# The first expert's rows gathered by token number, and its two products ahead of the end of the scatters

## The reference

```python
x = attn_out.transpose(0, 2, 1, 3).reshape(B * S, H * D)   # 2304 tokens x 512
do_compute = (x @ w_skip) > 0
xc = x[do_compute]
logits = xc @ w_gate                                       # 8 experts
e_idx = np.argmax(logits, axis=1)
gate_w = softmax(logits)[np.arange(len(xc)), e_idx]
for e in range(8):
    mask = e_idx == e
    h = np.maximum(xc[mask] @ w1[e], 0.0)                  # 512 -> 1024
    y[mask] = gate_w[mask, None] * (h @ w2[e])             # 1024 -> 512
out[do_compute] = xc + y
h = out @ w_in                                             # 512 -> 2048
g = where(h >= 1, h, where(h <= -1, 0, (h + 1)**2 / 4))
return g @ w_out                                           # 2048 -> 512
```

## Time and profile before

| | us |
|---|---|
| median of 3 runs | 693.38 |
| lowest, highest | 689.04, 693.66 |
| the profiled execution, device time | 696.19 |
| its span from first to last instruction | 694.3 |
| busy: TensorE, DVE, ACT, POOL | 639.6, 313.7, 188.2, 126.8 |

### The profile page before, as it was taken

One profiled execution on the slowest core, in us unless ns is written; L12 is line 12 of the kernel. 1 busy time (PEld: TensorE's weight loads), 2 busy tenths in 40 slices (PEclk: granted clock), 3 DMA queues, 4 the chain that ended last, 5 costly groups with the idle time before them and its releaser, 6 DMA issues.

```text
span 694.3 us, 12370 instructions
## 1 busy us (share of the span) xinstructions
PE 639.6 (92%) x5133; PEld 552.5 (80%) x5133; DVE 313.7 (45%) x570; ACT 188.2 (27%) x361; POOL 126.8 (18%) x135
## 2 busy tenths in 40 slices
PE   6888880699999999899999999999999999999995
PEld 3766660599999999788888888888888888888994
DVE  3766250051212111575545555456554565545652
ACT  1545450141111111122223322233222332223331
POOL 1333117002222223883000200002000020000201
PEclk8999695699999999999999999999999999999998
DMA  8687295883777885231000100001000010000100
GB/s 272 199 272 243 95 363 214 291 305 110 261 266 270 276 277 187 78 107 30 1 1 0 61 1 0 1 0 60 0 0 0 0 60 0 0 0 1 61 1 31
DMA packets 39476, 76.34 MB, mean 110 GB/s; under 512 B 3079, under 2 KB 17844, under 8 KB 38916
## 3 DMA queue, kind: packets, MB, share of 16 engines
q1 hardware_dynamic: 36556, 66.26, 27.9%
q0 software_dynamic: 2880, 9.52, 3.6%
HBM read 65.83 MB, written 9.94 MB: 109 GB/s over the span
## 4 chain that ended last, share of the span: by engine, by line
PE 86%; issue 4%; DMA 4%; DVE 3%; SPq 2%; POOL 1%; ACT 0%; DVEq 0%
PE pair L1025 28%; PE pair L1038 16%; PE bank L1038 13%; PE pair L982 11%; PE out_pair L992 5%; PE bank L992 5%; DMA k_loc<-kT 2%; PE out_pair L884 2%; PE pair L842 2%; PE bank L862 1%; PE out_pair L923 1%; DMA k_str<-kT 1%; DVE yl L780 1%; PE bank L966 1%; PE pair L836 1%
## 5 line engine op out<-in xcount | busy, mean ns | idle before, releaser
L1025 PE MATMUL pair<-yh,WIH 128*128 128x512 f32 (+1 forms) x320 | 116.7, 371 | 0.2 <-ACT yh L589 0.2
L1025 PE MATMUL pair<-yh,WIL 128*128 128x512 f32 (+1 forms) x320 | 116.6, 371 | 0.0
L613 ACT ACTIVATE cl<-cl,half 128x512 f32<-128x512 f32 (+1 forms) x80 | 54.4, 681 | 186.8 <-DVE cl L801 186.8
L809 DVE TENSOR_TENSOR gl<-gr,gh 128x512 fp32r<-128x512 f32 (+1 forms) x80 | 54.1, 677 | 73.6 <-ACT gh L622 73.2
L801 DVE TENSOR_SCALAR cl<-pair 128x512 f32<-128x512 f32 (+1 forms) x80 | 51.0, 637 | 72.9 <-PE pair L1025 72.9
L508 POOL DMA_INDIRECT out<-XT,tok x18 | 19.2, 1066 | 351.0 <-DVE XT L789 347.0
L1025 PE MATMUL pair<-yl,WIH 128*128 128x512 f32 (+1 forms) x320 | 79.6, 369 | 1.7 <-DVE yl L780 1.7
L982 PE MATMUL pair<-xw,WE 128*128 128x168 f32 x512 | 75.5, 309 | 0.0
L982 PEld LDWEIGHTS pair<-xw,WE 128*128 128x128 f32 x512 | 74.4, 192 | 0.1
L622 ACT CAST gh<-gr 128x512 fp32r<-128x512 f32 (+1 forms) x80 | 46.3, 579 | 86.1 <-PE bank L1038 61.0
L1025 PEld LDWEIGHTS pair<-yh,WIH 128*128 128x128 f32 x320 | 60.6, 189 | 11.3 <-ACT yh L589 0.6
(11 more groups left out here) (142 smaller groups left out, 804.8 us busy)
## 6 DMA issues: line engine op xcount, KB each, us to landing
WE<-w SPq DMA_DIRECT2D x16, 2048.0 KB, 10.0
xrow<-x_sorted SPq DMA_DIRECT2D x6, 781.5 KB, 9.7
v_loc<-vl SPq DMA_DIRECT2D x4, 1024.0 KB, 7.5
raw_in<-win SPq DMA_DIRECT2D x16, 256.0 KB, 8.5
raw_out<-wout SPq DMA_DIRECT2D x16, 256.0 KB, 2.6
q_loc<-qT SPq DMA_DIRECT2D x4, 576.0 KB, 6.4
k_loc<-kT SPq DMA_DIRECT2D x4, 576.0 KB, 7.8
v_str<-vs SPq DMA_DIRECT2D x8, 256.0 KB, 4.6
```

The lines of the kernel that those rows point to most:

```text
L613: act.activation(cl[:, 0:n], cl[:, 0:n], ACT.Square, bias=half[:, :], scale=0.5).then_inc(squared, 1)
L809: dve.tensor_tensor(gl[:, f % 2, 0:n], gr[:, 0:n], gh[:, f % 2, 0:n].bitcast(F32), ALU.subtract).then_inc(g_low, 1)
L1025: last = pe.matmul(h2_b[f % 2][:, 0:tokens], w[:, c, P * f:P * (f + 1)], x[:, c, 0:tokens], start=(k == 0), stop=(k == 3 * DC - 1))
```

## The change

The rows of `xrow` are also written to HBM unsorted (`x_tokens`), by nine transfers from SP of two tiles each, as ACT finishes the tiles. DVE builds for each of the 18 tiles a table `hot`: for each of its tokens a 1 at the slot that the token has, among slots 0 to 167. TensorE multiplies these tables by the tile number and the row number of each token (36 small matmuls), which gives for each slot the token that belongs there; DVE makes of them `token_of`. POOL, after its first 4 scatters (`SCATTERS_FIRST`), waits until all nine writes are done (`rows_out`), gathers the first expert's 168 rows from `x_tokens` with two indirect transfers, and goes on with the other 14 scatters. SP loads only expert 1's rows from `x_sorted`.

`into(0)` and `outof(0)` now both stand ahead of the wait for expert 1's rows, and `into(1)` ahead of the sort. The result of expert 0 is copied out of PSUM by DVE (`y_first`), since the banks are needed. Expert 0's w1 is loaded before the last steps of attention (the attention tiles were moved to the other end of the shared space), and expert 1's w1 after the nine writes.

```diff
@@ sync @@
-            sp.wait_ge(pv_done, STEPS)
             load_w1(0, 0)
+            sp.wait_ge(pv_done, STEPS)
             load_w2(0, 0)
+            for t in range(0, NT, ROWS_OUT):
+                sp.wait_ge(rows_copied, t + ROWS_OUT)
+                sp.dma_start(xt[P * t:P * (t + ROWS_OUT)].rearrange("(t p) c -> p t c", p=P), xrow[:, t:t + ROWS_OUT, 0:D]).then_inc(rows_out, 16)
             load_w1(1, 1)
...
             sp.wait_ge(scattered, 16 * NT)
-            for par in range(2):
-                sp.dma_start(xfirst[:, 2 * par, :], xs[bass.ds(start_1 if par else 0, P), 0:D]).then_inc(first_in[par], 16)
-                sp.dma_start(xfirst[0:WIN - P, 2 * par + 1, :], xs[bass.ds(start_1 + P if par else P, WIN - P), 0:D]).then_inc(first_in[par], 16)
-
+            sp.dma_start(xfirst[:, 2, :], xs[bass.ds(start_1, P), 0:D]).then_inc(first_in[1], 16)
+            sp.dma_start(xfirst[0:WIN - P, 3, :], xs[bass.ds(start_1 + P, WIN - P), 0:D]).then_inc(first_in[1], 16)
+
+            sp.wait_ge(rows_out, 16 * (NT // ROWS_OUT))
@@ gpsimd @@
             for t in range(NT):
+                if t == SCATTERS_FIRST:
+
+                    pool.wait_ge(rows_out, 16 * (NT // ROWS_OUT))
+                    for r, rows_ in ((0, P), (1, WIN - P)):
+                        pool.wait_ge(tokens_ready, r + 1)
+                        pool.indirect_dma_start(xfirst[0:rows_, r, :], None, xt, bass.IndirectOffsetOnAxis(token_of[0:rows_, r:r + 1], 0)).then_inc(first_in[0], 16)
                 pool.wait_ge(rows_copied, t + 1)
@@ vector @@
+            dve.wait_ge(slot_f_in, 16)
+            dve.tensor_copy(slot_b[:, :], slot_f[:, :]).then_inc(slot_b_ready, 1)
...
             dve.tensor_copy(slot_of[:, :], posf[:, :]).then_inc(slots_ready, 1)
+
+            dve.wait_ge(slot_b_ready, 1)
+            for t in range(NT):
+                dve.tensor_scalar(hot[:, t, :], slot_b[:, 0:WIN], posf[:, t:t + 1], None, ALU.is_equal).then_inc(hot_ready, 1)
             link(dve.tensor_copy(starts[:, :], base[0:1, :, 0]))
             dve.sem_inc(starts_ready, 1)
+            for r, rows_ in ((0, P), (1, WIN - P)):
+                dve.wait_ge(token_ready, r + 1)
+                dve.tensor_copy(token_parts[0:rows_, r, :], token_b[r][0:rows_, 0:2]).then_inc(token_copied, 1)
+                dve.wait_ge(token_copied, r + 1)
+                dve.scalar_tensor_tensor(token_of[0:rows_, r:r + 1], token_parts[0:rows_, r, 0:1], float(P), token_parts[0:rows_, r, 1:2], ALU.mult, ALU.add).then_inc(tokens_ready, 1)
...
-                dve.tensor_copy(xw[:, par, :, 0:P], first_b[2 * par][:, :].rearrange("p (c n) -> p c n", c=DC)).then_inc(first_main, 1)
+                dve.tensor_copy(xw[:, par, :, 0:P], first_b[0][:, :].rearrange("p (c n) -> p c n", c=DC)).then_inc(first_main, 1)
+                if par == 0:
+
+                    for c in range(DC):
+                        dve.wait_ge(y_ready, c + 1)
+                        dve.tensor_copy(y_first[:, c, :], y_b[c][:, 0:WIN]).then_inc(y_kept, 1)
@@ tensor @@
+            for r, rows_ in ((0, P), (1, WIN - P)):
+                for t in range(NT):
+                    if r == 0:
+                        pe.wait_ge(hot_ready, t + 1)
+                    last = pe.matmul(token_b[r][0:rows_, 0:2], hot[:, t, P * r:P * r + rows_], slot_b[:, WIN + 2 * t:WIN + 2 * t + 2], start=(t == 0), stop=(t == NT - 1))
+                last.then_inc(token_ready, 1)
...
+            first_rows(0)
             into(0, 0, 0, 1)
+            pe.wait_ge(tokens_ready, 2)
+            outof(0, 0, 1)
+            first_rows(1)
+            into(1, 1, 1, 1)
             sort_turned()
-            into(1, 1, 1, 1)
 
             pe.wait_ge(xt_dve, NT // 2)
             pe.wait_ge(xt_act, NT // 2)
-            outof(0, 0, 1)
-            for e in range(2, E):
+            outof(1, 1, 1)
+            into(2, 0, 2, 2)
+            for e in range(3, E):
                 into(e, e % 2, e % BUFS, e // 2 + 1)
                 outof(e - 1, (e - 1) % 2, (e - 1) // 2 + 1)
```

More of the change, by code:

```diff
@@ L95 @@
 LGW = 32
+ROWS_OUT = 2
+SCATTERS_FIRST = 4
 MASKS = 5
@@ L225, in program @@
         hid_b, y_b = bank[0:2], bank[2:6]
-        first_b, sort_b = bank[2:6], bank[2:6]
+        first_b, sort_b = bank[2:4], bank[2:6]
+        token_b = bank[4:6]
         h2_b, fin_b = bank[6:8], bank[0:4]
+        xt = nc.dram_tensor("x_tokens", (N, D), F32, kind="Internal").ap()
         xs = nc.dram_tensor("x_sorted", (XCOLS, ROW), F32, kind="Internal").ap()
@@ L559, in _, with place_first @@
             act.wait_ge(more_ready, 1)
-            for par in range(2):
+            def place_first(par):
                 act.wait_ge(first_turned, 2 * par + 2)
-                act.copy(xw[:, par, :, P:WIN], first_b[2 * par + 1][:, 0:DC * (WIN - P)].rearrange("p (c n) -> p c n", c=DC)).then_inc(first_rest, 1)
+                act.copy(xw[:, par, :, P:WIN], first_b[1][:, 0:DC * (WIN - P)].rearrange("p (c n) -> p c n", c=DC)).then_inc(first_rest, 1)
             def relus(e, par):
@@ L570, in relus @@
                     act.activation(hid[:, par, f, :], hid_b[f % 2][:, 0:WIN], ACT.Relu).then_inc(h_done, 1)
-            relus(0, 0)
+            for e in range(2):
+                place_first(e)
+                relus(e, e)
             for t in range(1, NT, 2):
@@ L577, in _ @@
             more_n = act.value_load(n_more[0:1, 0:1], min_val=0, max_val=EXTRA)
-            for e in range(1, E):
+            for e in range(2, E):
                 relus(e, e % 2)
@@ L759, in add @@
                     n = DC * e + c
-                    dve.wait_ge(y_ready, n + 1)
-                    dve.tensor_tensor(ytmp[:, c % 2, :], y_b[c][:, 0:WIN], gb[:, par, :], ALU.mult).then_inc(y_scaled, 1)
+                    if isinstance(e, int) and e == 0:
+                        dve.wait_ge(y_kept, c + 1)
+                        y = y_first[:, c, :]
+                    else:
+                        dve.wait_ge(y_ready, n + 1)
+                        y = y_b[c][:, 0:WIN]
+                    dve.tensor_tensor(ytmp[:, c % 2, :], y, gb[:, par, :], ALU.mult).then_inc(y_scaled, 1)
                     dve.wait_ge(y_scaled, n + 1)
@@ L987, in outof @@
                 for c in range(DC):
-                    behind(pe, y_scaled, DC * (e - 1) + c + 1)
+                    if not (isinstance(e, int) and e == 1):
+                        behind(pe, y_scaled, DC * (e - 1) + c + 1)
                     for f in range(FEC):
```

35 lines of the change are left out of this document (27 added, 8 removed).

## The result

| | before | changed |
|---|---|---|
| median of the runs, us | 692.29 (4 runs) | 702.48 (4 runs) |
| lowest, highest | 689.04, 693.66 | 700.98, 705.95 |
| the profiled execution, its span | 696.19, 694.3 | 705.95, 703.8 |

The ratio is 1.016, with a 95% interval of 1.0113 to 1.0207: 10 us slower, where 688.6 was forecast. Profile against profile it is 9.8 slower, and the forecast said 4.8 faster, so 14.6 us have to be found. A profile is of one execution: that of the kernel before took 3.9 us more than its median of 692.3, that of the changed kernel 3.5 more.

The account below looks back on a forecast made before the run. TensorE bounds the kernel, and POOL's scatter issuing its largest idle stretch. A gain of 13.1 us, less 6.1 of stall and 2.2 of clock, gives 4.8: from 693.38 to 688.6, own range 685 to 692, 8 in 10 680 to 694.

Parts of the forecast that it names:

- TensorE's start: At expert 0's gathered rows: TensorE starts at 114.2 us, 13.4 us before 127.65.
- into(0): Expert 0's first product: 10.41 us before, taken as 10.7 since it starts 1.5 us nearer to TensorE's first work.
- turning, into(1), sort: Behind outof(0): turning and copying expert 1's rows 1.5 us, into(1) 9.12, sort 9.82, ending at 156.6.
- stall for w1 of expert 3: Ahead of into(3): weights land 24.3 us behind the sort, wanted at 18.2, so TensorE idles 6.1 us.
- clock behind the stall: In into(3): half clock for 4.2 to 5.9 us costs 2.1 to 2.9 us; 2.2 taken.
- C: Rival, 12%: completions slow under load, 1.6 us in place of 0.5 at rows_out and the gather; 2.8 us less, 690.6.
- D: Rival, 13%: writes of x_tokens slow; at 225 GB/s rows_out comes at 120.3, and the time is 699.4, slower than before.
- 0.5 for completion: At rows_out: 0.5 us from the end of the writes' traffic to the waiting engine, as behind the last scatter.
- The rule against the change: HBM access takes 2 us at high load: rows_out and the gather each up to 1.8 us later, gain 1.2.
- The order of the work: Expert 1's rows at 134.5 precede outof(0)'s end at 136.1, so no wait; the rows_out wait covers DVE's tables.
- B: Rival, 13%: the stall before into(3) ends with most of its work at full clock; 7.0 us less, 686.4.
- A: Rival, 12%: w1 of expert 3 arrives in time, with no stall or clock fall; 13.1 us less, 680.3.

Follow-up runs that it names:

- e3: The changed kernel with all 18 scatters issued ahead of the two gathers: 707.71 us, ratio 1.0216.
- e1: The changed kernel once more, unaltered: 702.3 us, ratio 1.0155.
- e7: The kernel before, with ten scatters of 2084-byte rows to a spare tensor issued by POOL beside into(0): 698.59 us, ratio 1.0097.
- e4: The changed kernel with expert 0's eight relus on DVE in place of ACT: 702.02 us.
- after_same_chip: The changed kernel unaltered, a third time, on the chip of the fourth set: 698.06 us, ratio 1.0088.
- e13_same_chip: The changed kernel with w1 of expert 1 loaded only when the first gather has landed, run together with after_same_chip: 693.02 us, ratio 0.9992.
- e6: e2 with nine scatters in place of four ahead of the gathers: 691.67 us, ratio 0.9987.
- e9: e6 with SP's load of expert 1's w1 held until the first gather has landed: 682.04 us, ratio 0.9873; repeated on a fourth chip, 684.48, 0.9872.
- e2: The changed kernel with w1 of expert 3 issued as soon as expert 1's relus are done: 693.39 us, ratio 1.002.
- e10: e6 with three memsets, each waited for, ahead of each later scatter on POOL: 689.53 us, ratio 0.9984.
- e12: The kernel before, with 24 plain writes of 128 rows of 64 bytes by POOL beside the first product: 694.78 us, ratio 1.0035.
- e14: e2 with the load of expert 1's w1 held until the first gather has landed: 684.18 us, ratio 0.9866.
- e6_again: e6 unaltered, one run on a fourth chip: 687.7 us.

## Why the prediction was wrong

The terms of the sum, forecast against the first profile of the changed kernel, in us that the measured one is longer:

```
TensorE's start          114.2 -> 117.12     +2.9
into(0)                   10.7 -> 18.7       +8.0
outof(0)                   9.1 -> 9.7        +0.6
turning, into(1), sort    20.5 -> 21.2       +0.7
stall for w1 of expert 3   6.1 -> 7.0        +0.9
clock behind the stall     2.2 -> 3.3        +1.1
                                    sum     +14.2 of 14.6
```

**The step that failed** is "`into(0)` took 10.41 ..., so 10.7". It carried a duration from a place where POOL was idle to one where POOL issues scatters and their data moves, and asked only about the clock. e3 (no scatters beside it: 12.1 us for the 17.8 of e1) and e7 (scatters put beside it in the kernel before: 16.0 for 10.3) show that where signals come late the place costs it some 6 us, and e4 that it does so on DVE as on ACT. In after_same_chip the same place costs nothing: the term there is 11.0. No rival held this. C, slow completions, had the right shape (a signal behind its work) but looked at DMA's signals, and at 2 us.

**The start** was 2.9 late, 1.1 of it at `rows_out`: POOL was released at 110.58, not 109.5. The rate was right: the traffic went at 354 to 383 GB/s from 95 to 107 us, where 385 was taken, and the last packet of the writes ended at 108.8, where 109.1 was forecast. So D did not come. What was wrong is the 0.5 for completion, which measured 1.8. (The recorded 109.5 also drops 0.1: 109.1 and 0.5 are 109.6.) The other 1.8 is the gather, which took 4.3 us from the end of its issue to TensorE, against 2.5. There "0.5 more since w1 of expert 1 fills the DMA engines" was wrong: on the fourth chip the whole took 3.9 with that load ahead (after_same_chip) and 2.1 with it behind the gather (e13_same_chip), so the load costs 1.8. With nine scatters ahead of the gather as well it took 7.4 (e6) against 3.4 (e9).

**The rule against the change, and rival C.** C had 1.6 us in place of 0.5 at `rows_out` and at the gather. At `rows_out` it was right: 1.8 us, with the DMA engines at full share. At the gather it was not: its last packet ended at 116.5 and TensorE started at 117.12, 0.6 later, with the engines as full (0.99 to 1.05). Behind the last scatter, at a share of about 0.6, it was the 0.5 that the forecast had. The Trainium skill (DMA: Bandwidth & Descriptors, "Latency and other measured facts") puts HBM access at 2 us at high load. The trace agrees with it for the writes to HBM, and not for the gather, which writes into SBUF.

**The order of the work** held: expert 1's rows came in time, nothing was waited for between `outof(0)` and `into(1)`, the tables on DVE were hidden by the wait for `rows_out` (0.19 us each, the token numbers ready at 105.6), and the stall stood where it was forecast. e2 shows that it and its clock were worth 9 us. They were priced at 8.3 and measured 10.2 in the first profile; the clock came back only 6.1 us after work began, at 200.5. The prediction had taken 4.2 to 5.9 us for that. Both were read a little off: by the shares in the earlier trace rows the clock was back at 297.3 and not 297.7 (0.87 of the window from 297), and at 133.4 and not 133.6 (0.79 of the window from 133), so 3.8 and 5.8. B, the stall without a fall of the clock, was wrong: the clock was 0.53 in the idle window from 190 and 0.50 until 198. It fell at 190.2, 2.9 us after TensorE's last work, where the row that B leant on had 5.1. A, no stall, is what e2 made by hand.

**What is left.** Without late signals, and counted from the slots, the changed kernel ends 0.4 us behind the one before (595.3 and 594.9), where 4.8 ahead was forecast: start +3.1, `into(0)` +0.3, the rest until S +1.0, the stall and the clock +1.4 make 5.8, where 5.2 is seen. By the medians it is 5.9 behind on that chip. Most of that difference is the choice of the profiled executions: that of the kernel before took 3.9 us more than the median of its runs (696.2), that of after_same_chip 2.0 less than its own (696.0). The second group of its times stays open.

Open too is what makes TensorE's signals late. In the first profile and on the chips of sets 1 and 2 relus were late in all six kernels that had large scatters beside the product or just ahead of it, on two engines, and on the chips of sets 3 to 5 in none of eight profiles with such scatters. The last late relus start 1.9 to 3.3 us behind the end of POOL's last scatter issue, in all seven profiles, and what follows is on time. The token numbers say the same, in code that all these kernels share: the seven profiles of the first group that have them (e3 among them) show both of their signals 1.1 us or more behind TensorE's last matmul, the eight others 0.04. The second of them came 2.1 to 2.2 us behind where POOL paused after its first four scatters, and 6.3 and 7.8 where it went on scattering (e3, e6).

So large scatters beside TensorE's work are needed and not sufficient; the second condition is not in the programs. That it is the chip is argued and not shown. Each of the first three chips was used in one set only, so chip and moment are not told apart. Just two programs were profiled in both groups, a single execution in the second. It is not ACT, nor the instruction load, and in the first profile the DMA engines were not full (0.45 to 0.69), though in e7 they were (1.03). Whether the bytes, the indices or the unbroken issuing of the scatters matter is open as well, since e10 to e12 ran where no signal was late.

**Both kernels are beaten** by e9 and e14, at 0.987 of the time before: early rows pay when the w1 that they meet later is ordered early too (9 us) and the load beside the gather late. Both were measured only where no signal was late.

## What to carry to other kernels

When work is moved into a stretch where another engine is busy with DMAs, a duration taken from a quiet stretch is no more than a lower bound; price the handshakes between engines in it apart, above all where two buffers leave one signal of slack. When a start is pulled forward, follow each load behind it to its issue: here w1 of expert 3 sat behind steps that didn't matter, and moving one issue gave back 9 us, where the whole change was to bring 4.8. And compare variants that differ by a few us in one set on one chip, with the unaltered kernel among them, since one program read as two here. e9 looked like the effect of its one wait until e6_again and after_same_chip ran. When a time between traffic and a waiting engine is taken from a row, take it from a transfer of the same kind under the same load.

## What was not expected of the hardware

- A waiting, idle engine took up TensorE's result up to 7.8 us after the matmuls had ended by the profile: 3.5 and 4.6 us for relus of the changed kernel, 7.8 for `token_parts` in e6, against 0.04 otherwise. Waits that fall into that time end together. The profile can mark it as "remote" or "another core", on one core.
- The same program (e6) ended 3.4 us sooner in another set, 1.9 of it by S, and the changed kernel 9.6, 8.4 of it by S. What lies behind S in these differences has no account.
- A gather of 168 rows was in TensorE's hands 2.1 us after its issue, 3.9 with a 2 MB load ahead of it, 7.4 with that and a run of scatters ahead in its queue.
- The wait for nine writes to HBM ended 1.8 us after their last packet, with the DMA engines full; behind the last scatter it was 0.5, behind the gather 0.6.
- Behind a wait of 7.0 us the clock stayed at 0.50 for 6.1 us of full work, and `into(3)` took 12.4 us for 9.12.
